# A two-layer feed-forward kernel: the operands of the last product change sides

## The reference, cut to what matters

```python
sig = 1.0 / (1.0 + np.exp(-f_logit))
f = lower_bound + (1.0 - lower_bound) * sig          # (2, 6080, 256)
for t in range(S):
    h = f[:, t] * h + (1 - f)[:, t] * x[:, t]
    y[:, t] = h
x = y.reshape(B * S, D)                              # (12160, 256)
h = np.maximum(x @ w_in1, 0.0)                       # 256 -> 2048
z = h * h @ w_out1                                   # 2048 -> 256
h = z @ w_in2
g = np.where(h > 0.0, h, np.exp(np.minimum(h, 0.0)) - 1.0)
out = g @ w_out2                                     # 2048 -> 256
```

## Time and profile before

| | |
|---|---|
| median of 3 runs | 2102.45 us (2102.44 to 2103.11) |
| the profiled execution's own time | 2103.11 us |
| its span, first to last instruction | 2101.3 us |
| TensorE matmul busy | 2073.3 us, 9216 matmuls |
| TensorE weight load busy | 1725.4 us, 9216 loads |
| VectorE busy | 1200.7 us |
| ScalarE busy | 1204.3 us |
| GpSimd busy | 48.3 us |

### The profile page before, as it was taken

One profiled execution on the slowest core, in us unless ns is written; L12 is line 12 of the kernel. 1 busy time (PEld: TensorE's weight loads), 2 busy tenths in 40 slices (PEclk: granted clock), 3 DMA queues, 4 the chain that ended last, 5 costly groups with the idle time before them and its releaser, 6 DMA issues.

```text
span 2101.3 us, 28406 instructions
## 1 busy us (share of the span) xinstructions
PE 2073.3 (99%) x9216; PEld 1725.4 (82%) x9216; DVE 1200.7 (57%) x1928; ACT 1204.3 (57%) x2020; POOL 48.3 (2%) x40
## 2 busy tenths in 40 slices
PE   6999999999999999999999999999999999999998
PEld 5788888888888888888888888888888888888887
DVE  7955646556465564655646556455564655645544
ACT  4465655655556555565555655656556565565655
POOL 4400000000000000000000000000000000000000
PEclk9999999999999999999999999999999999999999
DMA  4411001010010100100101001010010100100000
GB/s 123 95 25 31 21 10 30 1 29 20 10 30 4 26 20 10 30 8 22 24 6 30 12 18 27 2 30 16 14 30 0 30 20 10 25 0 10 1 11 18
DMA packets 179101, 46.15 MB, mean 22 GB/s; under 512 B 172928, under 2 KB 179072, under 8 KB 179072
## 3 DMA queue, kind: packets, MB, share of 16 engines
q1 hardware_dynamic: 178944, 45.79, 9.7%
q0 software_dynamic: 128, 0.00, 0.0%
HBM read 33.29 MB, written 12.45 MB: 22 GB/s over the span
## 4 chain that ended last, share of the span: by engine, by line
PE 96%; DVE 2%; issue 1%; SPq 0%; ACT 0%; DMA 0%; POOL 0%; DVEq 0%; ACTq 0%
PE acc L258 48%; PE up L258 48%; SPq L186 0%; DVE y L514 0%; DVE hid_hi L560 0%; DVE gate L498 0%; DVE x_t L506 0%; DVE x_t L480 0%; DVE win_hi L475 0%; DMA x_raw<-in_x_dram 0%; DVE hid_lo L562 0%; DVE gate L480 0%; DVE wout L475 0%; ACT hid_hi L442 0%; POOL win_lo L641 0%
## 5 line engine op out<-in xcount | busy, mean ns | idle before, releaser
L258 PE MATMUL acc<-hid_hi,wout 128*128 128x512 f32 (+1 forms) x3072 | 1063.5, 387 | 3.3 <-DVE hid_lo L562 2.9
L258 PEld LDWEIGHTS acc<-hid_hi,wout 128*128 128x128 f32 x3072 | 576.3, 188 | 120.1 <-DVE hid_lo L562 4.5
L258 PE MATMUL acc<-hid_lo,wout 128*128 128x512 f32 (+1 forms) x1536 | 594.1, 387 | 0.0
L585 DVE TENSOR_TENSOR hid_lo<-hid,hid_hi 128x512 fp32r<-128x512 f32 (+1 forms) x384 | 263.7, 687 | 519.2 <-ACT hid_hi L442 519.2
L403 ACT ACTIVATE half<-up 128x512 f32<-128x512 f32 (+1 forms) x384 | 227.4, 592 | 439.9 <-PE up L258 439.6
L430 ACT ACTIVATE half<-up 128x512 f32<-128x512 f32 (+1 forms) x384 | 227.9, 593 | 356.4 <-PE up L258 356.2
L258 PEld LDWEIGHTS acc<-hid_lo,wout 128*128 128x128 f32 x1536 | 288.4, 188 | 57.1
L560 DVE CAST hid_hi<-hid 128x512 fp32r<-128x512 f32 (+1 forms) x384 | 160.2, 417 | 304.5 <-ACT hid L413 304.5
L258 PE MATMUL up<-y_hi,win_lo 128*128 128x512 f32 (+1 forms) x800 | 308.9, 386 | 18.3 <-DVE y_lo L527 17.9
L258 PE MATMUL up<-y_lo,win_hi 128*128 128x512 f32 (+1 forms) x800 | 308.5, 386 | 0.0
L258 PE MATMUL up<-y_hi,win_hi 128*128 128x512 f32 (+1 forms) x800 | 308.2, 385 | 0.0
(11 more groups left out here) (32 smaller groups left out, 837.4 us busy)
## 6 DMA issues: line engine op xcount, KB each, us to landing
f_raw<-in_f_logit_dram SPq DMA_DIRECT2D x184, 64.0 KB, 2.0
x_raw<-in_x_dram SPq DMA_DIRECT2D x184, 64.0 KB, 2.0
out_dram<-o_sb SPq DMA_DIRECT2D x184, 64.0 KB, 1.7
stage<-in_moe_w_in_dram SPq DMA_DIRECT2D x32, 64.0 KB
stage<-in_moe_w_out_dram SPq DMA_DIRECT2D x8, 256.0 KB
stage<-in_moe_w_in_dram SPq DMA_DIRECT2D x8, 256.0 KB
stage<-in_moe_w_out_dram SPq DMA_DIRECT2D x32, 64.0 KB
f_raw<-in_f_logit_dram SPq DMA_DIRECT2D x8, 48.0 KB, 1.9
```

The costliest lines, as they stand in the source:

```text
L258: mm = nc.tensor.matmul(out_ap, lhs[a], rhs[b], start=start and t == 0, stop=stop and t == 2)
L585: nc.vector.tensor_tensor(hid_lo[:, (j - 1) % RING, 0:N], hid[:, (j - 1) % 2, 0:N], hid_hi[:, (j - 1) % RING, 0:N].bitcast(F32), ALU.subtr ...
```

## The change

In `down2_chunk` the two operands change sides. The stationary operand becomes a 128 x 128 tile of `hid_hi` or `hid_lo` (128 hidden features by 128 tokens), and the moving operand the rows of `wout[1]`, whose hi and lo parts (256 + 256 columns) lie side by side. Per tile of 128 tokens there are two matmuls: `hid_hi` with 512 columns (hi and lo part at once) and `hid_lo` with 256 columns (the hi part alone). A full block has 4 such tiles, the tail 3. `acc2` now has tokens on the partitions, and for each tile 256 sums of the hi columns and 256 of the "cross" product `hid_hi` x `w_lo`; it takes four PSUM banks. The two halves have to be added: ScalarE copies the cross halves into `o_sb` (`copy_cross`, two instructions per block, at steps 3 and 4 of phase 1), and VectorE adds the other halves to them (`add_halves`, two per block, at steps 8 and 9). The transposition is gone, the output is stored in 2 DMAs per block with rows of 256 features (1 KB), and `w_out2` is loaded as it lies, in one DMA per chunk. For the tail, a semaphore after the second of the three tiles lets the copy of the first part begin, and each tile is stored by its own DMAs, 4 in all.

```diff
-        o_sb = sb("o_sb", [P, BANK // SQ, CH, SQ])
+        o_sb = sb("o_sb", [P, BANK // P, D])
-        acc2 = psum("acc2", [P, CH, BANK])
+        acc2 = psum("acc2", [P, BANK // P, 2, D])
+        def tiles(S_):
+            return range(B * S_ // P)
...
-                if kind == "out" and m == 1:
-                    for jj in range(J_PER_CHUNK):
-                        for cc in range(CH):
-                            sp.dma_start(dst[:, jj, cc * P:(cc + 1) * P].rearrange("p (a e) -> p a e", e=SQ),
-                                         wout2_v[:, c * J_PER_CHUNK + jj, :, cc, :]).then_inc(
-                                w_loaded[k % SLOTS], DMA_INC)
-                elif kind == "out":
-                    sp.dma_start(dst, wout1_v[:, c * J_PER_CHUNK:(c + 1) * J_PER_CHUNK, :]).then_inc(
+                if kind == "out":
+                    sp.dma_start(dst, wout_v[m][:, c * J_PER_CHUNK:(c + 1) * J_PER_CHUNK, :]).then_inc(
                         w_loaded[k % SLOTS], DMA_INC * G)
...
+                sp.wait_ge(out_evacuated, 2 * n + 2)
+                per = S // P
                 for b in range(B):
-                    for a in range(G):
-                        rows = out_v[b, bass.ds(n * S, S_), a * ROWRUN:(a + 1) * ROWRUN]
-                        i = o_sb[a * SQ:(a + 1) * SQ, b * per:(b + 1) * per, :, :]
-                        sp.dma_start(rows.rearrange("(k t) e -> t k e", t=SQ),
-                                     i.rearrange("t k c e -> t k (c e)")).then_inc(out_stored, DMA_INC)
+                    sp.dma_start(out_v[b, bass.ds(n * S, S), :].rearrange("(q p) d -> p q d", p=P),
+                                 o_sb[:, b * per:(b + 1) * per, :]).then_inc(out_stored, DMA_INC)
...
+            pieces = 0
+            for q in tiles(S_TAIL):
+                sp.wait_ge(out_evacuated, 2 * TAIL + q // 2 + 1)
+                col = q * P
+                while col < (q + 1) * P:
+                    b, s = divmod(col, S_TAIL)
+                    n = min((q + 1) * P - col, S_TAIL - s)
+                    p0 = col - q * P
+                    sp.dma_start(out_v[b, TAIL * S + s:TAIL * S + s + n, :],
+                                 o_sb[p0:p0 + n, q, :]).then_inc(out_stored, DMA_INC)
+                    pieces += 1
+                    col += n
...
                 elif j == 0:
-                    pe.wait_ge(out_evacuated, n)
-                for c in range(CH):
-                    mm = products(acc2[:, c, 0:N], [wout[1][:, j, h, c * P:(c + 1) * P] for h in range(2)],
-                                  [h[:, j % RING, 0:N] for h in (hid_hi, hid_lo)], j == 0, j == FC - 1)
+                    pe.wait_ge(out_evacuated, 2 * n)
+                for q in tiles(steps_of(n)):
+                    cols = slice(q * P, (q + 1) * P)
+                    nc.tensor.matmul(acc2[:, q, :, :], hid_hi[:, j % RING, cols], wout[1][:, j, :, :],
+                                     start=j == 0, stop=False, skip_group_check=True)
+                    mm = nc.tensor.matmul(acc2[:, q, 0, :], hid_lo[:, j % RING, cols], wout[1][:, j, 0, :],
+                                          start=False, stop=j == FC - 1, skip_group_check=True)
+                    if known(n, TAIL) and j == FC - 1 and q == 1:
+                        mm.then_inc(first_tiles_done, 1)
                 mm.then_inc(down2_done, 1)
...
+            def copy_cross(n, part):
+                if known(n, TAIL) and part == 0:
+                    act.wait_ge(first_tiles_done, 1)
+                else:
+                    act.wait_ge(down2_done, FC * (n + 1))
+                if part == 0:
+                    if not known(n, 0):
+                        act.wait_ge(out_stored, DMA_INC * B * n)
+                q1 = min(2 * part + 2, len(tiles(steps_of(n))))
+                nc.scalar.activation(o_sb[:, 2 * part:q1, :], acc2[:, 2 * part:q1, 1, :],
+                                     ACT.Copy).then_inc(cross_copied, 1)
...
+                    if j in (LAG, LAG + 1) and before is not None:
+                        copy_cross(before, j - LAG)
...
+                    if j == EARLY_UPS and before is None:
+                        for part in range(2):
+                            copy_cross(n - 1, part)
...
-            def evacuate(n):
-                N = B * steps_of(n)
-                dve.wait_ge(down2_done, FC * (n + 1))
-                if not known(n, 0):
-                    dve.wait_ge(out_stored, DMA_INC * B * G * n)
-                nc.vector.transpose(
-                    o_sb[:, 0:N // SQ, :, :].rearrange("p k c e -> p c k e"),
-                    acc2[:, :, 0:N].rearrange("p c (k e) -> p c k e", e=SQ)).then_inc(out_evacuated, 1)
+            def add_halves(n, part):
+                q1 = min(2 * part + 2, len(tiles(steps_of(n))))
+                dve.wait_ge(cross_copied, 2 * n + part + 1)
+                nc.vector.tensor_tensor(o_sb[:, 2 * part:q1, :], o_sb[:, 2 * part:q1, :],
+                                        acc2[:, 2 * part:q1, 0, :], ALU.add).then_inc(out_evacuated, 1)
...
-                    if j == ADD_STEP and before is not None:
-                        evacuate(before)
+                    if j in (ADD_STEP, ADD_STEP + 1) and before is not None:
+                        add_halves(before, j - ADD_STEP)
```

More of the change, by code:

```diff
@@ L148, in gated_scan_two_ffn @@
         hid2_lo_done = sem("hid2_lo_done")
+        first_tiles_done = sem("first_tiles_done")
+        cross_copied = sem("cross_copied")
         out_evacuated = sem("out_evacuated")
@@ L174, in _ @@
             win2_v = w_in2.rearrange("(c p) f -> p c f", p=P)
-            wout1_v = w_out1.rearrange("(j p) d -> p j d", p=P)
-            wout2_v = w_out2.rearrange("(j p) (a c e) -> p j a c e", p=P, a=G, c=CH)
+            wout_v = [w.rearrange("(j p) d -> p j d", p=P) for w in (w_out1, w_out2)]
             out_v = out.rearrange("(b t) d -> b t d", b=B)
@@ L220, in store_block @@
             def store_block(n):
-                S_ = steps_of(n)
-                per = S_ // SQ
-                sp.wait_ge(out_evacuated, n + 1)
+                sp.wait_ge(out_evacuated, 2 * n + 2)
+                per = S // P
                 for b in range(B):
-                    for a in range(G):
-                        rows = out_v[b, bass.ds(n * S, S_), a * ROWRUN:(a + 1) * ROWRUN]
-                        i = o_sb[a * SQ:(a + 1) * SQ, b * per:(b + 1) * per, :, :]
-                        sp.dma_start(rows.rearrange("(k t) e -> t k e", t=SQ),
-                                     i.rearrange("t k c e -> t k (c e)")).then_inc(out_stored, DMA_INC)
+                    sp.dma_start(out_v[b, bass.ds(n * S, S), :].rearrange("(q p) d -> p q d", p=P),
+                                 o_sb[:, b * per:(b + 1) * per, :]).then_inc(out_stored, DMA_INC)
             load_rows(0, f_logit, f_raw, f_loaded)
@@ L247, in _ @@
                 store_block(n)
-            store_block(TAIL)
-            sp.wait_ge(out_stored, DMA_INC * B * G * N_BLOCKS)
+            pieces = 0
[10 more added lines that the diff above has]
+                    col += n
+            sp.wait_ge(out_stored, DMA_INC * (B * N_FULL + pieces))
         @block.tensor
@@ L467, in _ @@
             phase2(TAIL, None, None, False)
+            for part in range(2):
+                copy_cross(TAIL, part)
         @block.vector
@@ L580, in phase2 @@
                     if j == EARLY_UPS and before is None:
-                        evacuate(n - 1)
+                        for part in range(2):
+                            add_halves(n - 1, part)
                     c = FC * n + j
@@ L628, in _ @@
             phase2(TAIL, None, None, False)
-            evacuate(TAIL)
+            for part in range(2):
+                add_halves(TAIL, part)
         @block.gpsimd
```

## The result

The changed kernel takes 2125.27 us (median of 4 runs, 2125.15 to 2125.61) against 2102.48 us of the kernel before: ratio 1.0108, 95% interval [1.0094, 1.0122], so 22.8 us slower. The forecast was 2110.6 us, 8.2 us slower, with a range up to 2122 us. The direction was right, the size was not, and the time lies outside the range.

A forecast was written before the change was run, and what follows sets the result against it. TensorE, with 96% of the chain, was taken to bound the kernel. Its +9.8 us, +0.3 us at block 22 and -1.9 us at the end gave 2102.45 + 8.2 = 2110.6 us against the median, range 2100 to 2122 us.

The forecast's parts named there:

- part 1: TensorE's down chunks in full blocks: 8 matmuls instead of 6, same columns, 26.7 ns more per chunk, +9.8 us in all.
- The term of +9.8 us: TensorE's added time over 368 down chunks of the full blocks, 26.7 ns each; the tail's chunks add nothing.
- The 120 ns: Forecast cost of one 256-column matmul on TensorE, 106.7 + 13.3 ns, extrapolated from 384 and 512 columns.
- The judgement on the load: The next stationary operand's load, about 0.11 us, still hides behind a 256-column matmul, by some 10 ns.
- The load doesn't hide: Rival: loads behind 256-column matmuls take longer, 1.5 us more per ns, up to 2192 us; chance 0.15 from 2118 us up.
- The other three: Rivals: extra shrinks (2100.6 us, 0.13); short matmul without extra (2090.4 us, 0.06); ScalarE's copies show (about 2120 us, 0.04).
- Part 2: ScalarE's copies and VectorE's additions per full block fit into idle time: cost 0; uncovered copies up to 26 us.
- Part 3: Where block 22 is emptied: two copies ahead of the relu on ScalarE delay it, +0.3 us, bounds 0 and 1.2 us.
- Part 4: The end after the last matmul: four store issues instead of eight, T + 4.5 us instead of 6.4, -1.9 us.
- Part 5: The start: loading `w_out2` with 8 issues instead of 32, which neither VectorE nor TensorE waited for: 0.

## Why the prediction missed

**The step that failed** is in part 1: "In these stretches the cost is columns x 0.417 ns + 13.3 ns per matmul with its load." That held for streams of one length, and I applied it to a stream of two. The two lengths that I had measured stood in separate stretches. It gave +26.7 ns per step; measured were +66.7 ns.

The trace of the kernel before had the evidence. Where the tail's chunks meet those of block 22, five steps have 384s and 512s side by side, and the chain shows them (start us, us, what):

```profile
2017.88 1.39 PE up L258 x6
2019.27 1.05 PE acc L258 x6
2020.32 1.38 PE up L258 x6
...
2058.13 1.39 PE acc L258 x6
```

Six 512s take 1.38 to 1.39 us there, as in the changed kernel, and 1.36 us among their own kind; the three steps around 2018 us take 2.43 us each instead of the 2.40 us of the rule. So a missing term could be read before the change, though for another pair of lengths: 33 ns per return. The term of +9.8 us in the sum became, from TensorE's first start to its last end, (2118.30 - 17.25) - (2094.90 - 17.89) = +24.0 us. Of this 9.8 us are the two more matmuls per chunk, as worked out, and 14.2 us are left for the mixture; 368 x 40 ns would be 14.7 us, and of the 0.5 us between them 0.3 us are a shorter wait for `hid_lo` (2.6 us instead of 2.9).

**The 120 ns** for 256 columns was right for a row of short matmuls: 12 in a row take 1.43 us. Between long ones they take 113 to 120 ns. The judgement on the load was right too: with 24 short ones a step at 120 ns each no load shows. The rule of the Trainium skill, "TensorE: Matmul & The Clock Gate", section "LDWEIGHTS (loading the stationary operand)", columns / 1.2 in ns, gives 107 ns for 128 columns, and the runs agree with it. The same page's extra of about 2.5 ns per warm matmul (one at the full clock) (section "Wait — 56ns, not 53.3ns?") doesn't fit here: an estimate by it is 12 x (106.7 + 2.5) = 1310 ns for 12 of them, and they take 1430.

**The rivals.** "The load doesn't hide" was the one whose time fits (it began at 2118 us), but not its mechanism: the delay sits on the long matmuls behind the short ones. By its price list, 1.5 us for each ns on a short matmul, the total would be read as short matmuls of 130 ns, and in the trace's full blocks none takes more than 120 (mean 116). The other three fell.

**Part 2**, the elementwise work at 0: right. TensorE waits for neither, and the kernel with the lengths alone loses the same per step. **Part 3**, +0.3 us: 0. By the forecast the copies start 0.9 us ahead of the end of the up matmuls and take 1.2 us; they start 1.0 us ahead of it (2085.42 us) and take 1.09 us together. **Part 4**, -1.9 us: -1.2 us. The addition and the first issue come as forecast, 1.0 us behind TensorE; but four issues take 2.21 us, 0.55 us each and not 0.46, and 2.5 us and not 2.1 us pass from the start of the last issue to the end. **Part 5**, 0: TensorE's first matmul comes 0.6 us earlier, at 17.25 us. Over the traces it lies between 17.3 and 17.9 us in the eight with the old loads of `w_out2`, and between 17.2 and 17.4 us in the seven with the new ones, so the 0.6 us is within the scatter of the old ones; whether the new loads give a part of it isn't shown. The profiled execution before is itself 0.6 us above the median of its runs. The measured terms, 24.0 - 0.6 - 1.2 = 22.2 us, make up the difference of the spans; without the 0.6 us they are the 22.8 us between the medians.

**What stays open** is the mechanism of the 20 ns. The runs show a net delay that comes with the order of the matmuls' lengths, also with the old operands and without any new work of other engines (the kernel with the lengths alone), and also where down chunks take the place of up chunks (short ones first). No row shows what is being waited for.

## What to carry to other kernels

When TensorE holds the whole chain, as here, cutting the same columns into more matmuls costs twice: once per matmul (13.3 ns here), and once more where shorter ones stand in a stream of long ones. Keep the lengths of a stream equal, or put the short ones next to each other (four together cost 20 ns, four between long ones 40 ns). A cost per instruction that is read off stretches of one kind is good for such stretches; for a mixture, look first for a place in the old trace where the kinds already stand side by side (here steps of 2.43 us instead of 2.40), and else widen the range by a price per change of kind. And an instruction mix can slow code that the change doesn't touch, so compare the untouched groups too (here the up chunk, 1.36 to 1.39 us).

## What the runs showed of the hardware

- A matmul of fp32r with its own load costs its columns at 2.4 GHz plus 13.3 ns in streams of one length: 120.0 ns for 256, 173.3 for 384 and 226.7 for 512.
- Behind two or more of 256 columns, 512-column matmuls take up to 9 ns more than 226.7 ns each, for five matmuls; then the distance is 226.7 ns again. The first two of the 256s take 7.5 ns less together, so the net loss is 20 ns. Behind eight of 384 columns the loss was 33 ns, more than behind twelve of 256, and all but one of the six long ones took 229 to 235 ns.
- With two single 256s among eleven 512s, steps with the same matmuls took 2750, 2777 and 2800 ns in turn.
- Which operand is stationary and which is streamed made no difference of a nanosecond (2786.7 ns a step either way). With eight 512s in a down chunk and swapped sides a step took the nominal 3173.3 ns.
- Where the edits cut the tail's chunks of 384 columns into halves of 192, the rule of columns and 13.3 ns (93.3 ns) no longer holds even for a pair: with two short ones per chunk the first took 88 ns, the second 110 and the 384 behind them 198 instead of 173.
- Two DMA queues issued four stores each in 1.8 and 1.9 us side by side, where one took 3.7 us for eight.
